# Odd pairs' solve results placed in the other block's PSUM rows

## The chip, the cores and the metric

The kernel runs on one core of one Trainium2 chip. The metric is the device time of one execution in microseconds (us). The core has a matrix engine (TensorE, PE in the profile; its loads of weights are PEld), VectorE (DVE), ScalarE (ACT), GpSimd (POOL), and a sync engine (SP) that issues all the DMA transfers. Results of PE go to PSUM, a small memory of 128 partitions, from which DVE and ACT read them.

## The reference

Two parts follow each other: a recurrent attention over 768 steps for 4 x 8 heads of size 40, and on its output two feed-forward layers.

```
for t in range(S):
    y[:, :, t] = einsum('bhd,bhde->bhe', rt, state)
    Sa = einsum('bhde,bhe->bhd', state, at)
    state = state * wt[:, :, None, :] - einsum('bhd,bhe->bhde', Sa, bt)
    state = state + einsum('bhd,bhe->bhde', vt, kt)
x = y as (3072, 320)
x = ((x @ w1) * (x @ w2)) @ w3 @ w_out        # 320 -> 1024 -> 1024 -> 320
out = (maximum(x @ w_in, 0) ** 2) @ w_out2    # 320 -> 2048 -> 320
```

All is float32.

## The kernel before

**Windows.** The recurrence is cut into chunks of 64 tokens, and within a chunk it becomes matrix algebra. A window n handles one chunk for two of the four batches, 16 heads, so there are 24 windows; even and odd windows belong to different batches. The 16 heads of a window are 8 pairs x (X = 8), and a pair has two heads q = 0 and 1. Head q lies on partitions 64q to 64q + 63 of most tiles.

**The solve.** Within a chunk each token's correction depends on the earlier ones, which is a triangular system of 64 unknown rows per head. It is split in two blocks of BLK = 32 rows. The inverses of the 32x32 diagonal blocks are worked out by POOL, in 31 steps of a multiplication and an addition for all heads at once (`invert`, L660 to L676), and turned by DVE (`turn_inverse`). Then, on PE: `make_u0` (L772) multiplies block 0's inverse with its right-hand side `x_row`; ACT copies the result from PSUM into `uv` (`copy_u`, L1193); `make_x1` (L785) multiplies the block below the diagonal (`n10`) with it; DVE adds the product to block 1 of `x_row` (`add_x1`, L1489); `make_u1` (L798) multiplies block 1's inverse with that; ACT copies again. `turn_uv` (L802) then transposes the complete `uv`.

`make_u0` and `make_u1` both go through `solve_block` (L764). Each batch goes over the 8 pairs and for every x over both q: 16 float32 matmuls, of which the profile lists each twice, as 32. A matmul there has 32 rows, 32 columns of weights and 40 moving columns. The rows of the PE array that it uses follow from the partitions of its operands, the columns from the partitions in PSUM to which its result goes. Results for pair x lie in columns 40x to 40x + 39 of `its_first(n)`, the first half of the PSUM tile `both` (in odd windows of the opening: `aside`), on partitions 64q + 32 at to 64q + 32 at + 31 for block `at`.

**Other steps of a window.** `turn_w`, `turn_ar`, `turn_bk`, `turn_rows` and `turn_uv` are transposes on PE; `cross` (L727), `make_z` (L747), `add_state` (L814), `make_read` (L823), `make_y` (L834) and `turn_state` (L848) are matmuls with up to 128 rows. After each, ACT or DVE takes the result out: `copy_x` and `copy_rows` on ACT, `scan`, `invert_decay` (a reciprocal in two halves), `mask_ak`, `mask_read` and `scale_y` on DVE.

**The experts.** The feed-forward layers run over 6 tiles of 512 tokens. `w3 @ w_out` is multiplied once in the opening (`turn_w3`, `multiply_w3`, on PE between the windows' steps). Weights and activations are split in a high and a low part (`h_hi`, `h_lo`, `x_hi`, `x_lo`), which PE multiplies in 8 terms of 128x512 (`into_hidden`, L866), and in `fold` (L938) and `project` (L953) to the output. For each hidden tile ACT copies one half (`take`), DVE multiplies (`combine`, L1556 or L1558), ACT rounds to `h_hi` (L1250), DVE subtracts to `h_lo` (L1548), and PE awaits `lo_made` before it uses that tile and before it overwrites a bank.

**The order.** It is written out by hand for each engine, with semaphores between them. Windows 0 to 3 (OPENING = 4) lie in an opening that interleaves several windows with the `w3` product. From window 4 on, each engine runs a loop over the windows in which every `next(beside)` stands for one step of the experts; a window has 14 of them, and 56 steps make an expert tile, so that four windows stand beside one expert tile. On PE the order around the change is: `make_u0(n)`, an expert step, `turn_rows(n + 1)`, an expert step, `turn_w(n + 2)`, `make_x1(n)`, an expert step, `make_u1(n)`, an expert step, `turn_uv(n)`. The experts' x of tile i is read back from DRAM (`load_x`) after y of four windows was stored there (`store_y`). After window 23 the last experts run alone.

Of the kernel before, what the change touches and what calls it, by code (L numbers as in the profile page):

```python
# [7 lines left out]
ALU = mybir.AluOpType  # L8
# [69 lines left out]
def attention_with_experts(nc, xT_dram, inputs, w1, w2, w3, w_out, w_in, w_out2, out):  # L78


    P, C, X, DP = 128, inputs.C, inputs.PAIRS, 64
    B, H, S, D = inputs.r.shape
    E = DP + D
    BLK = 32
# [29 lines left out]
    with ExitStack() as ctx:  # L114
        def sb(name, shape, dt=F32):
            return ctx.enter_context(nc.sbuf_tensor(name, shape, dt))
# [4 lines left out]
        w_raw, ar_raw, bk_raw, uv, zv = inputs.w_raw, inputs.ar_raw, inputs.bk_raw, inputs.uv, inputs.zv  # L121
# [14 lines left out]
        invT = [sb(f"invT{h}", [P, X, BLK]) for h in range(2)]  # L136
        x_row = [sb(f"x_row{h}", [P, X, D]) for h in range(2)]
# [79 lines left out]
        def its_both(n):  # L217
            return (aside if n < OPENING and n % 2 else both)[:]

        def its_first(n):  # L220
            return its_both(n)[:, 0:512]
# [10 lines left out]

        def by_head(bank, rows, cols=D):
            return bank[rows, 0:X * cols].rearrange("t (x d) -> t x d", x=X)

        def rbd_of(n):
            return spare[n - 2] if 2 <= n < OPENING else rbd[n % 2]
# [448 lines left out]
        def _(pe):  # L686
# [77 lines left out]
            def solve_block(n, at, signal):  # L764
                for x in range(X):
                    for q in range(2):
                        rows = slice(DP * q + BLK * at, DP * q + BLK * (at + 1))
                        last = nc.tensor.matmul(its_first(n)[rows, x * D:(x + 1) * D], invT[n % 2][rows, x, :], x_row[n % 2][rows, x, :],  # L768
                                                start=True, stop=True)
                last.then_inc(signal, 1)  # L770

            def make_u0(n):  # L772
                pe.wait_ge(inverse_turned, n + 1)
                pe.wait_ge(x_copied, n + 1)
                if n < OPENING - 1:
                    pe.wait_ge(masked_ak, 2 * (n + 3))
                    pe.wait_ge(blocks_copied, 2 * (n + 3))
                elif OPENING <= n and n + 1 < WINDOWS:
                    pe.wait_ge(masked_ak, 2 * (n + 2))
                    pe.wait_ge(blocks_copied, 2 * (n + 2))  # L780
                elif n + 1 == WINDOWS:
                    pe.wait_ge(y_scaled, n)
                solve_block(n, 0, u0_made)

            def make_x1(n):  # L785
                half = n % 2
                pe.wait_ge(u0_copied, n + 1)
                if OPENING <= n and n + 1 < WINDOWS:
                    pe.wait_ge(rows_copied, n + 2)
                for x in range(X):  # L790
                    for q in range(2):
                        lo = DP * q
                        last = nc.tensor.matmul(its_first(n)[lo + BLK:lo + DP, x * D:(x + 1) * D],  # L793
                                                n10[n % 4][lo:lo + BLK, x, :], uv[half][lo:lo + BLK, x, q, 0:D],
                                                start=True, stop=True)
                last.then_inc(x1_made, 1)

            def make_u1(n):  # L798
                pe.wait_ge(x1_added, n + 1)
                solve_block(n, 1, u1_made)  # L800
# [245 lines left out]
            make_u0(0)  # L1046
            turn_ar(3)
            make_x1(0)
            multiply_w3(2, 2)
            multiply_w3(3, 1)  # L1050
# [14 lines left out]
            make_u0(1)  # L1065
            turn_rows(2)
            make_x1(1)
            make_z(2)
            turn_w(4)
# [14 lines left out]
            turn_w(5)  # L1084
            make_z(3)
            make_x1(2)
            multiply_w3(5, 0)
            make_u1(2)
# [73 lines left out]
        def _(act):  # L1162
# [26 lines left out]
            def copy_x(n):  # L1189
                act.wait_ge(z_made, n + 1)  # L1190
                nc.scalar.copy(x_row[n % 2][:], by_head(its_z(n), slice(0, P))).then_inc(x_copied, 1)

            def copy_u(n, at, made, copied):  # L1193
                act.wait_ge(made, n + 1)
                for q in range(2):
                    rows = slice(DP * q + BLK * at, DP * q + BLK * (at + 1))
                    last = nc.scalar.copy(uv[n % 2][rows, :, q, 0:D], by_head(its_first(n), rows))  # L1197
                last.then_inc(copied, 1)

            def reset(n):  # L1200
# [17 lines left out]
            def copy_state(n):  # L1218
                act.wait_ge(turned_state, n + 1)
                nc.scalar.copy(st[n % 2][0:E], by_head(its_second(n), slice(0, E))).then_inc(st_copied, 1)  # L1220
# [98 lines left out]
            for c in range(4):  # L1319
                rows = slice(BLK * c, BLK * (c + 1))  # L1320
                last = nc.scalar.copy(unit_rows[rows], ident[rows, rows].rearrange("i (x r) -> i x r", r=4).unsqueeze(
                    3).broadcast_to([BLK, X, 4, X]))
# [20 lines left out]
            copy_w3(3)  # L1343
            copy_blocks(2)
            copy_u(0, 0, u0_made, u0_copied)
            copy_r(3)
            copy_u(0, 1, u1_made, u1_copied)
            round_fold(2)
            copy_uvT(0)
# [4 lines left out]
            copy_w3(5)  # L1354
            copy_state(0)
            copy_u(1, 0, u0_made, u0_copied)
            copy_rows(2)
            round_split(0)
# [67 lines left out]
        def _(dve):  # L1426
# [62 lines left out]
            def add_x1(n):  # L1489
                dve.wait_ge(x1_made, n + 1)  # L1490
                for q in range(2):
                    rows = slice(DP * q + BLK, DP * (q + 1))
                    last = nc.vector.tensor_tensor(x_row[n % 2][rows], by_head(its_first(n), rows), x_row[n % 2][rows],
                                                   ALU.add)
                last.then_inc(x1_added, 1)

            def new_state(n):
# [153 lines left out]
            fill_lanes(2)  # L1651
            scale_a(3)
            add_x1(0)
            invert_decay(3, 0)
            invert_decay(3, 1)
# [7 lines left out]
            fill_lanes(3)  # L1663
            scale_y(0)
            add_x1(1)
            rest_of_split(0)
            scan(4)
# [9 lines left out]
            fill_lanes(4)  # L1677
            scan(5)
            add_x1(2)
            rest_of_fold(4)  # L1680
            invert_decay(5, 0)
# [57 lines left out]
def attention_then_experts(nc, r, k, v, w, a, b, w1, w2, w3, w_out, w_in, w_out2, out):  # L1739
    B, H, S, D = r.shape  # L1740

    xT_dram = nc.dram_tensor("xT", (H * D, B * S), F32, kind="Internal").ap()
    with ExitStack() as ctx:
        inputs = Inputs(nc, ctx, r, k, v, w, a, b)
        attention_with_experts(nc, xT_dram, inputs, w1, w2, w3, w_out, w_in, w_out2, out)
# [22 lines left out]
```

## Time and profile before

| | us |
|---|---|
| median of 3 runs | 1058.69 (1058.61 to 1059.34) |
| profiled execution | 1060.74 |
| its span | 1059.0 |
| PE busy | 1023.2 (97%) |
| PE, loads of weights | 880.8 (83%) |
| DVE busy | 634.7 (60%) |
| POOL busy | 486.1 (46%) |
| ACT busy | 419.7 (40%) |

The busy times are those of one profiled execution. Loads of weights overlap matmuls. A matmul's end is modelled, so a batch of matmuls overlaps the first one after it by up to 0.2 us in the listing; the starts are what to go by. Times in the text count from the start of the span. The granted clock of PE is full for most of the span, and lower in two stretches before 120 us.

### The profile page before, as it was taken

The page shows a single profiled execution, that of the slowest core. Times are in us where ns is not written, and L with a number is a line of the kernel's source. Part 1 is how long each engine was busy: PE and PEld are TensorE (multiplying, and loading weights), DVE is VectorE, ACT ScalarE, POOL GpSimd, SP SyncE. Part 2 cuts the span into 40 slices and gives each one's busy share as a digit, 9 for nine tenths or more (in the row PEclk, how much of TensorE's full clock was granted, in tenths as well). Part 3 has the DMA queues.
Part 4 walks back from the last instruction along what each step waited for, and adds up shares of the span by engine and source line. Part 5 has one row for each costly group of instructions (what it writes and reads, how often), then busy time and mean ns, then how long its engine had stood idle before and what let it go on. Part 6 is the DMA issues. An engine that isn't in the chain of part 4 may idle for free.

```text
span 1059.0 us, 27606 instructions
## 1 busy us (share of the span) xinstructions
PE 1023.2 (97%) x11008; PEld 880.8 (83%) x11008; DVE 634.7 (60%) x1005; ACT 419.7 (40%) x796; POOL 486.1 (46%) x1573
## 2 busy tenths in 40 slices
PE   5998989999999999999999999999999999999998
PEld 5786768779898888898888898888988888897797
DVE  6876366777875656666567566467567555442333
ACT  3453434454543343443344343334434234332332
POOL 4777755527447346346346355355365364200000
PEclk8997999999999999999999999999999999999999
DMA  9953556756886764757665757756648744555552
GB/s 177 188 127 65 155 132 170 197 165 203 226 234 178 170 150 126 180 145 180 151 157 131 176 140 202 150 134 155 160 125 217 154 117 132 154 169 184 166 170 75
DMA packets 267390, 169.05 MB, mean 160 GB/s; under 512 B 199680, under 2 KB 229376, under 8 KB 267264
## 3 DMA queue, kind: packets, MB, share of 16 engines
q1 hardware_dynamic: 267264, 167.29, 62.7%
q8 instruction: 88, 1.44, 0.6%
q14 instruction: 38, 0.31, 0.1%
HBM read 141.03 MB, written 26.21 MB: 158 GB/s over the span
## 4 chain that ended last, share of the span: by engine, by line
PE 79%; DVE 4%; ACT 2%; issue 1%; ACTq 0%; DVEq 0%
PE aside L866 31%; PE moe_bank L953 16%; PE moe_bank L938 8%; PE both L830 3%; PE both L730 3%; PE both L768 3%; PE both L840 2%; PE both L844 2%; PE both L760 2%; PE both L811 2%; PE both L743 1%; PE both L819 1%; PE both L793 1%; PE both L853 1%; PE both L716 1%
## 5 line engine op out<-in xcount | busy, mean ns | idle before, releaser
L671 POOL TENSOR_TENSOR inv_tmp<-blk,inv 128x60 f32<-128x60 f32 (+24 forms) x744 | 209.5, 282 | 358.4 <-DVE blk L1480 301.4
L675 POOL TENSOR_TENSOR inv<-inv,inv_tmp 128x60 f32<-128x60 f32 (+24 forms) x744 | 237.4, 319 | 58.3
L953 PE MATMUL moe_bank<-v_ring,h_hi 128*128 128x320 f32 x768 | 175.3, 315 | 0.0
L866 PE MATMUL aside<-x2T_hi,w_ring 128*128 128x512 f32 x480 | 148.0, 405 | 4.4 <-DVE h_lo L1548 4.3
L866 PE MATMUL aside<-xT_hi,w_ring 128*128 128x512 f32 x480 | 148.2, 406 | 2.2 <-DVE h_lo L1548 1.5
L1558 DVE SCALAR_TENSOR_TENSOR aside<-aside,left 128x512 f32<-128x512 f32 x96 | 66.9, 697 | 122.0 <-ACT left L1258 122.0
L953 PEld LDWEIGHTS moe_bank<-v_ring,h_hi 128*128 128x128 f32 x768 | 128.0, 188 | 3.9
L1548 DVE TENSOR_TENSOR h_lo<-aside,h_hi 128x512 fp32r<-128x512 f32 x144 | 97.4, 677 | 49.7 <-ACT h_hi L1250 49.0
L1250 ACT CAST h_hi<-aside 128x512 fp32r<-128x512 f32 x144 | 84.7, 588 | 94.9 <-DVE aside L1558 49.6
L953 PE MATMUL moe_bank<-v_ring,h_lo 128*128 128x320 f32 x384 | 118.6, 309 | 0.0
L1258 ACT ACTIVATE left<-aside 128x512 f32<-128x512 f32 x96 | 57.4, 598 | 117.3 <-PE aside L866 117.3
L866 PEld LDWEIGHTS aside<-x2T_hi,w_ring 128*128 128x128 f32 x480 | 84.1, 188 | 21.3 <-issue 6.3
L866 PEld LDWEIGHTS aside<-xT_hi,w_ring 128*128 128x128 f32 x480 | 84.7, 188 | 19.2 <-DVE h_lo L1548 2.6
L866 PE MATMUL aside<-xT_lo,w_ring 128*128 128x512 f32 x288 | 97.1, 391 | 0.0
L866 PE MATMUL aside<-x2T_lo,w_ring 128*128 128x512 f32 x288 | 96.9, 391 | 0.0
L1438 DVE RECIPROCAL undecay<-decay 104x256 f32<-104x256 f32 x48 | 83.2, 1739 | 0.2
L938 PE MATMUL moe_bank<-h_hi,v_ring 128*128 128x512 f32 x240 | 81.4, 404 | 0.0
L953 PEld LDWEIGHTS moe_bank<-v_ring,h_lo 128*128 128x128 f32 x384 | 72.1, 188 | 0.0
L1556 DVE TENSOR_TENSOR aside<-left,aside 128x512 f32<-128x512 f32 x48 | 33.0, 687 | 63.1 <-PE aside L866 63.1
L866 PEld LDWEIGHTS aside<-xT_lo,w_ring 128*128 128x128 f32 x288 | 54.1, 188 | 12.8 <-DVE xT_lo L1564 0.6
L866 PEld LDWEIGHTS aside<-x2T_lo,w_ring 128*128 128x128 f32 x288 | 54.1, 188 | 12.3 <-DVE x2T_lo L1586 0.2
L1197 ACT COPY uv<-both 32x320 f32<-32x320 f32 x88 | 36.8, 418 | 68.9 <-PE both L768 63.4
(151 smaller groups left out, 1604.2 us busy)
## 6 DMA issues: line engine op xcount, KB each, us to landing
w_ring<-gate_rows SPq DMA_DIRECT2D x40, 640.0 KB, 4.6
w_ring<-win_rows SPq DMA_DIRECT2D x40, 640.0 KB, 4.1
v_ring<-wout_rows SPq DMA_DIRECT2D x80, 320.0 KB, 3.1
v_ring<-fold_rows SPq DMA_DIRECT2D x48, 320.0 KB, 4.2
gate_rows<-w_ring SPq DMA_DIRECT2D x8, 640.0 KB, 6.4
win_rows<-w_ring SPq DMA_DIRECT2D x8, 640.0 KB, 4.4
wout_rows<-v_ring SPq DMA_DIRECT2D x16, 320.0 KB, 5.9
stage<-in_moe_w SPq DMA_DIRECT2D x8, 512.0 KB
```

Source lines behind the costliest of these rows:

```text
L671: nc.gpsimd.tensor_tensor(tmp, x[:, j, 0:j].unsqueeze(2).broadcast_to([P, j, X - lo]), mine[:, j:j + 1, lo:X].broadcast_to([P, j, X - lo]) ...
L675: nc.gpsimd.tensor_tensor(mine[:, 0:j, lo:X], mine[:, 0:j, lo:X], tmp, ALU.add).then_inc(solve, 1)
L866: last = nc.tensor.matmul(bank(use), w, x, start=n == 0, stop=n == len(terms) - 1)
L938: last = nc.tensor.matmul(bank(f"x{m}"), weights[:, lo:lo + P], h[at % RING][:], start=f == 0 and n == 0, stop=f == FT - 1 and n == len(te ...
L953: last = nc.tensor.matmul(bank(f"o{s}")[:, 0:M], h[at % RING][:, s * P:(s + 1) * P], weights[:, rest * M:(rest + 1) * M], start=f == 0 and ...
L1197: last = nc.scalar.copy(uv[n % 2][rows, :, q, 0:D], by_head(its_first(n), rows))
L1250: nc.scalar.copy(h_hi[at % RING][:], hidden_at(x)).then_inc(hi_made, 1)
L1258: nc.scalar.activation(left[x % 2][:], hidden_at(x), ACT.Relu).then_inc(taken, 1)
L1438: nc.vector.reciprocal(undecay[0:E, xs], decay[n % 4][0:E, xs, 1:C + 1]).then_inc(undecayed, 1)
L1548: nc.vector.tensor_tensor(h_lo[at % RING][:], hidden_at(x), h_hi[at % RING][:].bitcast(F32), ALU.subtract).then_inc(lo_made, 1)
L1556: nc.vector.tensor_tensor(into, left[x % 2][:], into, ALU.mult).then_inc(combined, 1)
L1558: nc.vector.scalar_tensor_tensor(out=into, in0=into, scalar=0.0, in1=left[x % 2][:], op0=ALU.max, op1=ALU.mult).then_inc(combined, 1)
```

## The change

Results of the three batches for odd pairs (x odd) go to the other block's partitions in PSUM: for block `at`, to 64q + 32 (at ^ 1). Even pairs stay. Operands stay where they are. In PSUM, then, a block's results of even pairs and of odd pairs lie on different partitions, and each reader takes them in two instructions, one for the even and one for the odd pairs, each with half the pairs: `copy_u` on ACT has four copies of 32 x 160 for two of 32 x 320, `add_x1` on DVE four additions for two. The destination in `uv` and `x_row` is as before. Semaphores, waits and order don't change.

```diff
--- before.py
+++ after.py
@@ -232,6 +232,13 @@
 
         def by_head(bank, rows, cols=D):
             return bank[rows, 0:X * cols].rearrange("t (x d) -> t x d", x=X)
+
+        def solved_rows(q, at, odd):
+
+            return slice(DP * q + BLK * (at ^ odd), DP * q + BLK * ((at ^ odd) + 1))
+
+        def solved(n, q, at, odd):
+            return by_head(its_first(n), solved_rows(q, at, odd))[:, odd::2, :]
 
         def rbd_of(n):
             return spare[n - 2] if 2 <= n < OPENING else rbd[n % 2]
@@ -765,8 +772,8 @@
                 for x in range(X):
                     for q in range(2):
                         rows = slice(DP * q + BLK * at, DP * q + BLK * (at + 1))
-                        last = nc.tensor.matmul(its_first(n)[rows, x * D:(x + 1) * D], invT[n % 2][rows, x, :], x_row[n % 2][rows, x, :],
-                                                start=True, stop=True)
+                        last = nc.tensor.matmul(its_first(n)[solved_rows(q, at, x % 2), x * D:(x + 1) * D],
+                                                invT[n % 2][rows, x, :], x_row[n % 2][rows, x, :], start=True, stop=True)
                 last.then_inc(signal, 1)
 
             def make_u0(n):
@@ -790,7 +797,7 @@
                 for x in range(X):
                     for q in range(2):
                         lo = DP * q
-                        last = nc.tensor.matmul(its_first(n)[lo + BLK:lo + DP, x * D:(x + 1) * D],
+                        last = nc.tensor.matmul(its_first(n)[solved_rows(q, 1, x % 2), x * D:(x + 1) * D],
                                                 n10[n % 4][lo:lo + BLK, x, :], uv[half][lo:lo + BLK, x, q, 0:D],
                                                 start=True, stop=True)
                 last.then_inc(x1_made, 1)
@@ -1194,7 +1201,8 @@
                 act.wait_ge(made, n + 1)
                 for q in range(2):
                     rows = slice(DP * q + BLK * at, DP * q + BLK * (at + 1))
-                    last = nc.scalar.copy(uv[n % 2][rows, :, q, 0:D], by_head(its_first(n), rows))
+                    for odd in range(2):
+                        last = nc.scalar.copy(uv[n % 2][rows, odd::2, q, 0:D], solved(n, q, at, odd))
                 last.then_inc(copied, 1)
 
             def reset(n):
@@ -1490,8 +1498,9 @@
                 dve.wait_ge(x1_made, n + 1)
                 for q in range(2):
                     rows = slice(DP * q + BLK, DP * (q + 1))
-                    last = nc.vector.tensor_tensor(x_row[n % 2][rows], by_head(its_first(n), rows), x_row[n % 2][rows],
-                                                   ALU.add)
+                    for odd in range(2):
+                        mine = x_row[n % 2][rows, odd::2, :]
+                        last = nc.vector.tensor_tensor(mine, solved(n, q, 1, odd), mine, ALU.add)
                 last.then_inc(x1_added, 1)
 
             def new_state(n):
```

## Rows read from the trace of the kernel before

**Rows 1.** The page: busy time (share, instructions), and the chain by engine.
```profile
PE 1023.2 (97%) x11008; PEld 880.8 (83%) x11008; DVE 634.7 (60%) x1005; ACT 419.7 (40%) x796; POOL 486.1 (46%) x1573
...
PE 79%; DVE 4%; ACT 2%; issue 1%; ACTq 0%; DVEq 0%
```

**Rows 2.** Stretches: start:end, length, busy (instructions) of each engine, PE clock, DMA share, GB/s.
```profile
79.00:100.00 21.00, 16.04 (x256) 14.27 (x257) 13.89 (x19) 6.72 (x14) 16.56 (x57) 0.88 0.42 75
300.00:460.00 160.00, 159.51 (x1791) 138.72 (x1786) 100.34 (x158) 64.64 (x124) 78.69 (x261) 1.00 0.67 165
```

**Rows 3.** Timeline of PE in window 13: start, us, line, operation, count.
```profile
519.99 0.39 PE L866 MATMUL aside<-xT_lo,w_ring 128*128 128x512 f32 x1
520.31 0.76 PE L768 MATMUL both<-x_row,invT 32*32 32x40 f32 x32
521.00 0.50 PE L938 MATMUL moe_bank<-h_hi,v_ring 128*128 128x512 f32 x1
...
526.91 1.20 PE L866 MATMUL aside<-xT_hi,w_ring 128*128 128x512 f32 x4
...
528.95 0.76 PE L768 MATMUL both<-x_row,invT 32*32 32x40 f32 x32
```

**Rows 4.** Groups of PE: line, tile, shape, count, busy us, mean ns, idle before.
```profile
L830 PE MATMUL both<-rbd,uvT 104*128 104x128 f32 x352 | 42.9, 275 | 0.0
L768 PE MATMUL both<-x_row,invT 32*32 32x40 f32 x1408 | 34.6, 202 | 6.6 <-DVE azk L1471 6.3 <-DVE x_row L1493 0.3
...
L760 PE MATMUL both<-zv,azk 128*64 128x40 f32 x352 | 25.1, 233 | 0.9 <-ACT bk_row L1187 0.9
...
L853 PE MATMUL both<-ident,sT 104*40 104x40 f32 x640 | 15.7, 206 | 0.0
```

**Rows 5.** Timeline of PE, batches of other steps.
```profile
535.04 1.11 PE L760 MATMUL both<-zv,azk 128*64 128x40 f32 x32
...
538.03 1.95 PE L830 MATMUL both<-rbd,uvT 104*128 104x128 f32 x16
...
543.58 0.78 PE L853 MATMUL both<-ident,sT 104*40 104x40 f32 x32
```

**Rows 6.** Groups of ACT: copies by shape.
```profile
L1197 ACT COPY uv<-both 32x320 f32<-32x320 f32 x88 | 36.8, 418 | 68.9 <-PE both L768 63.4 <-issue 3.4
...
L1182 ACT COPY n<-both 32x256 f32<-32x256 f32 x44 | 16.0, 363 | 15.7 <-DVE azk L1471 15.4
...
L1284 ACT COPY third<-moe_bank 64x512 f32<-64x512 f32 x6 | 3.5, 585 | 13.0 <-PE moe_bank L938 13.0
```

**Rows 7.** Groups of DVE: additions and multiplications by shape.
```profile
L1471 DVE TENSOR_TENSOR azk<-both,above 64x512 f32<-64x512 f32 x44 | 30.3, 689 | 1.0
...
L1493 DVE TENSOR_TENSOR x_row<-both,x_row 32x320 f32<-32x320 f32 x44 | 21.6, 490 | 25.8 <-PE both L793 25.1
```

**Rows 8.** Timeline of DVE in window 16, from add_x1.
```profile
648.11 0.99 DVE L1493 TENSOR_TENSOR x_row<-both,x_row 32x320 f32<-32x320 f32 x2 [1.24 <-PE both L793]
...
651.19 1.74 DVE L1438 RECIPROCAL undecay<-decay 104x256 f32<-104x256 f32 x1
652.85 0.63 DVE L1548 TENSOR_TENSOR h_lo<-aside,h_hi 128x512 fp32r<-128x512 f32 x1
```

**Rows 9.** Timeline of PE in window 16, the expert step after turn_uv.
```profile
653.53 1.20 PE L866 MATMUL aside<-xT_hi,w_ring 128*128 128x512 f32 x4
```

**Rows 10.** Timeline of PE in the opening; idle time before it in brackets.
```profile
96.96 1.27 PE L768 MATMUL both<-x_row,invT 32*32 32x40 f32 x32 [4.29 <-DVE azk L1471]
```

**Rows 11.** Timeline of DVE in the opening.
```profile
93.72 0.67 DVE L1486 STREAM_TRANSPOSE invT<-inv 128x256 f32<-128x256 f32 x1 [4.71 <-POOL inv L675]
```

**Rows 12.** Groups of ACT between 118 and 146 us.
```profile
L1265 ACT CAST xT_hi<-x_raw 128x512 fp32r<-128x512 f32 x3 | 1.7, 618 | 4.3 <-DMA x_raw<-xT 4.3
```

## Prediction

> **What bounds the kernel now.** I read the page first: TensorE (PE) is busy 97% of the span and the chain that ended last is 79% PE [rows 1]. The table by stretch then says where this holds. From 300 us on PE is busy 159.51 of 160 us at full clock, with VectorE (DVE) at 100 and ScalarE (ACT) at 65; between 79 and 100 us it is busy only 16.04 of 21 us, at a mean clock of 0.88 [rows 2]. So a microsecond taken from PE's instructions in the steady stretch (windows 4 to 23) shortens the kernel, unless a wait takes its place; in the opening (windows 0 to 3) it may be lost to an idle stretch.
>
> The order of PE's work there shows what the change touches: a solve, then a step of the expert matmuls, which covers the reply of ACT or DVE [rows 3]. Each window has three such batches (two solves at L768, one product at L793), so 72 batches, 60 of them in windows 4 to 23. The code has 16 float32 matmuls in a batch and the profile 32; every one of them stands twice (as do the 8 of L830, listed as 16). "A matmul" below is such a record.
>
> **What one batch costs, and what sets it.** A batch runs from its first start to its last end in 0.76 us [rows 3]; one matmul lasts 202 ns in the mean [rows 4]. So 31 starts lie in about 0.56 us: one every 18.2 ns. Records of the two head parities q already lie in different tiles of the array (rows 0 and columns 0, rows 64 and columns 64). One tile thus gets a matmul every 36.4 ns. Is that the tile's own speed? The read step, a single stream of 128 columns, takes (1.95 - 0.275)/15 = 112 ns each, 0.87 ns a column [rows 4, 5]; 40 columns are then 35 ns. That fits 36.4, and it says that a tile streams at full speed and that the two tiles overlap completely. turn_state (L853) has 104 rows in both parities, so its two tiles share all rows and differ in columns alone, and its spacing is (0.78 - 0.206)/31 = 18.5 ns [rows 4, 5]: two column tiles over the same rows overlap as well as two disjoint ones. That is the case the change makes: even pairs keep their columns, odd pairs go to the other 32, and four column tiles are in use, each row group feeding two, as in L853.
>
> **PE, the gain.** If four overlap, each tile still takes 36.4 ns a matmul, now four per period: one start every 9.1 ns. The batch shrinks by 31 x 9.1 = 0.28 us; I take 0.27, since the first loads are exposed either way. Bounds: nothing (the spacing stays 18.2) to 0.28. Below nothing: if the load of weights into one column tile can't run beside a matmul of the neighbour on the same rows. make_z, with 64 weight columns and 40 moving ones, has (1.11 - 0.233)/31 = 28.3 ns [rows 4, 5], 57 ns in a tile, so a load costs 0.88 ns a column, 28 ns for 32 columns; exposed for each pair it would add 16 x 28 = 0.45 us to a batch (16 matmuls in each of the two tiles). I take a value near the upper end, because L853 and L760 overlap both loads and matmuls over shared rows. The number of PE instructions and their waits stay.
>
> The Trainium skill ("TensorE: Matmul & The Clock Gate", section "The mechanism") says that a weight load overlaps running matmuls only when the row group differs. L853's rows above disagree for two tiles of 64 columns; for neighbours of 32 columns no row shows it. By that rule the change would bring nothing on PE, and perhaps the loss just bounded. The same page ("Wait — 56ns, not 53.3ns?") states a least start-to-start of about 25 ns; the 18.2 ns of these rows are below it, so I don't let it bound the new spacing.
>
> **ACT and DVE, the cost.** copy_u becomes four copies of 32x160 for two of 32x320. 256 columns take 363 ns and 512 take 585 [rows 6], 0.87 ns a column; 160 columns come to 280. Extra: 4 x 280 - 2 x 418 = 0.28 us, twice a window. That the odd copy reads other partitions than it writes should cost nothing: the copy of L1284 reads rows 64 to 127 into 0 to 63 and is on this same line. add_x1: 512 columns 689 ns, 320 490 [rows 7], so 160 are 324, and four come to 0.32 us more than two. Between-instruction gaps are nearly nothing on both engines. Every-second-head reads could cost more; bounds: from 0.28 and 0.32 down to 0 and up to a doubling.
>
> Where are they covered? After x1 PE has an expert step of 2.04 us (526.91 to 528.95) before the second solve [rows 3], while add_x1 takes 0.99 us; 1.32 still fits. The same step covers copy_u. One place in four windows isn't covered. In windows 4, 8, 12, 16 and 20 DVE goes without a pause from add_x1 through the scan, a combine and a reciprocal to the h_lo that PE's next expert step awaits: 648.11 to 653.48 [rows 8], and PE starts at 653.53 [rows 9]. From x1 to there DVE sets the time. The gain of the second solve (0.27) is swallowed and 0.32 is added: 5 x 0.59 = 3.0 us. DVE's other chains start after cross or the state steps, far from add_x1. Windows 22 and 23, where DVE's combine comes late, and the crowded part before 300 us get an allowance of 1.0 us.
>
> **The opening.** PE idles 4.29 us before the first solve of window 2, and reports DVE's azk [rows 10]; DVE itself sat 4.71 us until the inverse from GpSimd (POOL) was there [rows 11]. POOL's chain of inversions doesn't change, so windows 0 and 1 gain nothing; their slower copies vanish in the same idle time. Window 2 then runs at half clock, 1.27 us a batch [rows 10], and would save about 0.5 three times. Window 3 saves 0.81 but has hardly any cover (one small multiply of 1.3 us): about 0.55 goes back. 1.5 + 0.3 = 1.8 us. They pass on, because the experts start when x is loaded from the y just stored (ACT waits 4.3 us on that DMA) [rows 12]. Bounds 0 to 3.
>
> **Sum.** 60 x 0.27 = 16.2; less 3.0; less 1.0; plus 1.8: 14.0 us. The profiled execution took 1060.74 us (span 1059.0), so 1046.7 in its terms; the median of the runs is 2.05 below it: 1044.7, rounded to 1045 (-1.3%).
>
> **The rivals.** *Half the overlap.* Something shared by the four (the supply of 64 loads and matmuls in 0.28 us, half the time it has now) stops the spacing near 13.6 ns. For: nothing in the trace runs denser than 18.2. Against: it would have to bind just below what is seen. The same terms as in the sum are then 60 x 0.14 - 5 x (0.14 + 0.32) - 0.7 + 1.0 = 6.4: 1052 us. Chance 0.14.
> *It doesn't do what it says.* Neighbouring columns on one row group take turns, PE is unchanged, and the longer add_x1 shows five times (1.6 us), in the opening about 1: 1061 us, on the edge of what can be told. Chance 0.13.
> *Slower: exposed weight loads.* The 0.45 us above in 72 batches, 32 us plus the 2.6: about 1093 us. It decides as soon as over 4 ns per matmul are added. Against: shared rows overlap in L853. Chance 0.05.
> *The forecast*, four tiles at once: 0.66, with its own range of 1040 to 1049. The last 0.02 is for a clock loss in the opening or unforeseen.
>
> **How the numbers follow.** About 0.2% (2 us) can be told from no change. Faster: 0.66 + 0.14 + a bit of the second rival = 0.81. Same: 0.08, from the second rival. Slower: 0.11, its other half and the third. The range reaches from all 72 batches gaining with few waits (1039) to past the half overlap: 1056.
>
> **What would show it.** L768 and L793 batches of about 0.49 us from first start to last end, for 0.76; PE's step from a solve to the next expert step 0.42 for 0.69; ACT's copies 280 ns, twice as many; DVE's adds 324 ns; a stall before the expert step after turn_uv in one window of four, with h_lo as its releaser; the idle time before 97 us longer by up to 1.6. Batches of 0.76 or more prove the forecast wrong; so do batches of 0.49 with new PE waits of over 5 us in the steady stretch.

## The result and the profile after

| | before | changed |
|---|---|---|
| median of 4 runs | 1058.76 us | 1046.43 us (1045.58 to 1049.25) |
| profiled execution, span | 1059.0 us | 1047.5 us |
| PE busy | 1023.2 us | 1005.5 us |
| ACT busy, instructions | 419.7 us, 796 | 432.0 us, 892 |
| DVE busy, instructions | 634.7 us, 1005 | 641.1 us, 1053 |

The ratio is 0.9882 (95% interval 0.9860 to 0.9904). Measured again in a later session, beside three of the experiments (run changed_again), it was 0.9888 (0.9868 to 0.9907; 1046.04 us for 1059.29). The forecast was 1045 us.

The page of the changed kernel, against [rows 1]:

```profile
span 1047.5 us, 27750 instructions
...
PE 1005.5 (96%) x11008; PEld 860.6 (82%) x11008; DVE 641.1 (61%) x1053; ACT 432.0 (41%) x892; POOL 485.4 (46%) x1573
...
PE 75%; DVE 7%; issue 2%; ACT 2%; ACTq 0%; DVEq 0%
```

PE lost 17.7 us of work, and its share of the chain that ended last went from 79% to 75%, DVE's from 4% to 7%. The stretch from 300 us, against [rows 2] (columns as there):

```profile
300.00:460.00 160.00, 159.12 (x1829) 137.80 (x1828) 102.26 (x167) 66.78 (x141) 78.84 (x262) 1.00 0.66 163
```

PE stays all but full, so what it saves there is time. PE's timeline in window 16, against [rows 3]:

```profile
633.91 0.39 PE L873 MATMUL aside<-xT_lo,w_ring 128*128 128x512 f32 x1
634.23 0.49 PE L775 MATMUL both<-x_row,invT 32*32 32x40 f32 x32
634.65 1.20 PE L873 MATMUL aside<-xT_hi,w_ring 128*128 128x512 f32 x4
...
639.87 0.49 PE L800 MATMUL both<-uv,n 32*32 32x40 f32 x32
640.28 1.19 PE L873 MATMUL aside<-xT_hi,w_ring 128*128 128x512 f32 x4
...
642.32 0.49 PE L775 MATMUL both<-x_row,invT 32*32 32x40 f32 x32
642.74 1.19 PE L873 MATMUL aside<-xT_hi,w_ring 128*128 128x512 f32 x4
...
644.70 1.03 PE L818 MATMUL both<-ident,uv 128*104 128x128 f32 x8
646.18 1.19 PE L873 MATMUL aside<-xT_hi,w_ring 128*128 128x512 f32 x4 [0.45 <-DVE h_lo L1557]
```

A batch lasts 0.49 us for 0.76, and from a solve's first start to the next expert step there are 0.42 us for 0.69. The last line carries what was lost: the expert step after turn_uv finds PE idle for 0.45 us, and names h_lo (by the starts it is 0.69 us late: 1.48 us after turn_uv, for 0.79 in the windows where nothing waits and 0.86 here in the kernel before). The groups of PE, against [rows 4]; one matmul lasts as long as before, so the whole gain is in how many run at once:

```profile
L775 PE MATMUL both<-x_row,invT 32*32 32x40 f32 x1408 | 22.2, 203 | 6.9 <-DVE azk L1479 5.0 <-DVE x_row L1503 1.9
...
L800 PE MATMUL both<-uv,n 32*32 32x40 f32 x704 | 11.0, 203 | 0.0
```

ACT's and DVE's new readers, against [rows 6] and [rows 7]:

```profile
L1205 ACT COPY uv<-both 32x160 f32<-32x160 f32 x176 | 49.7, 282 | 56.5 <-PE both L775 54.9
```

```profile
L1503 DVE TENSOR_TENSOR x_row<-both,x_row 32x160 f32<-32x160 f32 x88 | 28.3, 321 | 21.0 <-PE both L800 19.7
```

The steady stretch can be read off far more exactly than the total: the first solve of window 12 to that of window 16, which is one expert tile's period. Before it is 161.70 us (in the same timeline the starts are 479.69 and 641.39). The changed kernel:

```profile
475.17 0.49 PE L775 MATMUL both<-x_row,invT 32*32 32x40 f32 x32
...
634.23 0.49 PE L775 MATMUL both<-x_row,invT 32*32 32x40 f32 x32
```

159.06 us, 2.64 less, and the same in each later group of four windows, to 0.01 us. The experiments below are read by this period, since the totals scatter by several microseconds from chip to chip and run to run (24 runs of the kernel before on one chip lie between 1055.97 and 1063.6). What the starts are inside one batch is told in ns from the first (PE's records in one batch of L768 or L775; for each of the 16 matmuls two of them):

```
before : 0 6 52 59 93 100 129 136 165 ...          566   (565 or 566 in 46 of 48 batches, the others at half clock)
changed: 0 6 13 20 52 59 65 72 93 100 106 113 ...  292   (292 or 293 in 45 of 48, the others in the opening)
```

Two starts per period of 36 ns, 6 to 7 ns apart, have become four, 6.5 ns apart.

### The profile page after: what moved, and what is told of

Same layout as the page of the kernel before. It is cut to its first block, busy times and chain, and to the rows that moved or that the text cites. A ratio compares the mean times of both kernels' runs of the same rounds, so it can differ in the third digit from the quotient of the medians.

```text
span 1047.5 us, 27750 instructions
## 1 busy us (share of the span) xinstructions
PE 1005.5 (96%) x11008; PEld 860.6 (82%) x11008; DVE 641.1 (61%) x1053; ACT 432.0 (41%) x892; POOL 485.4 (46%) x1573
## 4 chain that ended last, share of the span: by engine, by line
PE 75%; DVE 7%; issue 2%; ACT 2%; ACTq 0%; DVEq 0%
PE aside L873 30%; PE moe_bank L960 15%; PE moe_bank L945 8%; PE both L837 3%; PE both L737 3%; PE both L847 2%; PE both L851 2%; PE both L767 2%; PE both L775 1%; PE both L826 1%; PE both L818 1%; PE both L750 1%; PE both L860 1%; PE both L723 1%; PE both L707 1%
## 5 line engine op out<-in xcount | busy, mean ns | idle before, releaser
L1205 ACT COPY uv<-both 32x160 f32<-32x160 f32 x176 | 49.7, 282 | 56.5 <-PE both L775 54.9
L873 PEld LDWEIGHTS aside<-x2T_lo,w_ring 128*128 128x128 f32 x288 | 54.1, 188 | 12.3 <-DVE x2T_lo L1595 0.2
```

The source lines that it names most:

```text
L873: last = nc.tensor.matmul(bank(use), w, x, start=n == 0, stop=n == len(terms) - 1)
L1205: last = nc.scalar.copy(uv[n % 2][rows, odd::2, q, 0:D], solved(n, q, at, odd))
```

## Experiments

The diffs are against the changed kernel, with lines left out.

**split_only.** Is it the overlap of column tiles, or do the split reads do something?

```diff
-            return slice(DP * q + BLK * (at ^ odd), DP * q + BLK * ((at ^ odd) + 1))
+            return slice(DP * q + BLK * at, DP * q + BLK * (at + 1))
```

> The readers are split in even and odd pairs as in the changed kernel (four copies of 32x160, four additions), but the results stay in their old PSUM rows. Theory (the gain is the overlap of four column tiles): batches stay at 0.76 us, PE gains nothing, only the cost of the split is left: h_lo later by 0.32 us in five windows (1.6 us) and about 1 us in the opening, so about 1061 us. Rival (the split itself frees something, or costs more than the sums say): 1050 or less, or 1064 or more.

Measured: 1060.86 us for 1061.06 of the kernel before on that chip, 0.9991 (0.9974 to 1.0008), so no difference against the kernel before on its own chip. The expected 1061 us was met in the number alone: it stood for a loss of 2.3 us, and the interval goes from 2.8 us faster to 0.8 slower, so a loss of that size is ruled out. The batches are 0.76 us:

```profile
477.54 0.76 PE L775 MATMUL both<-x_row,invT 32*32 32x40 f32 x32
...
639.41 0.76 PE L775 MATMUL both<-x_row,invT 32*32 32x40 f32 x32
```

The period is 161.87 us, 0.17 longer than before and not 0.32. The reason stands in add_x1, which took 1.14 us here and 1.33 in the changed kernel (next two fences, DVE's timelines in window 16, split_only and then the changed kernel):

```profile
646.12 1.14 DVE L1503 TENSOR_TENSOR x_row<-both,x_row 32x160 f32<-32x160 f32 x4 [1.24 <-PE both L800]
```

```profile
640.42 1.33 DVE L1503 TENSOR_TENSOR x_row<-both,x_row 32x160 f32<-32x160 f32 x4 [0.99 <-PE both L800]
641.78 1.56 DVE L1438 TENSOR_TENSOR_SCAN decay<-both,zeros 104x64 f32<-104x64 f32 x8
643.25 0.67 DVE L1565 TENSOR_TENSOR aside<-left,aside 128x512 f32<-128x512 f32 x1
643.84 1.74 DVE L1446 RECIPROCAL undecay<-decay 104x256 f32<-104x256 f32 x1
645.50 0.63 DVE L1557 TENSOR_TENSOR h_lo<-aside,h_hi 128x512 fp32r<-128x512 f32 x1
```

The instructions last the same, 318 and 320 ns in the median. But their starts differ (ns from the first; DVE's additions, ACT's copies):

```
split_only: DVE 0 245 564 819     ACT 0 190 481 675
changed:    DVE 0 330 657 1002    ACT 0 294 586 882
```

Where two instructions in a row read the same PSUM rows, the second starts 72 ns (DVE) or 93 ns (ACT) before the first ends. In the changed kernel each reads other rows than the last, and starts 12 to 14 ns after its end. So the split itself is cheaper than forecast, and the move of rows takes this back.

**evens_first, twos, evens3.** How far does PE look for a free tile? The three differ from the changed kernel in the order of pairs alone.

```diff
-                for x in range(X):
+                for x in [*range(0, X, 2), *range(1, X, 2)]:      # evens_first
+                for x in (0, 2, 1, 3, 4, 6, 5, 7):                # twos
+                for x in (0, 2, 4, 1, 3, 5, 6, 7):                # evens3
```

> As the changed kernel, but each batch runs over pairs 0, 2, 4, 6 and then 1, 3, 5, 7, so that the four column tiles are never asked for in turn. Theory A (matmuls start in program order and one whose tile is busy holds back all behind it): two tiles at a time, batches of 0.76 us, and the time of split_only, about 1061 us. Theory B (PE picks any matmul of its queue whose tile is free): batches of 0.49 us and 1046 us.

> As the changed kernel, with pairs in the order 0, 2, 1, 3, 4, 6, 5, 7. In evens_first the first odd pair started just when pair 4 did, with pair 6's two matmuls still waiting for their tiles: PE seems to look past one waiting pair (two matmuls), not past more. Theory (a look-ahead of one pair): pair 1 goes past the waiting pair 2, full overlap, batches of 0.49 us. Rival (a fixed time or a start-up effect, no look-ahead): pair 1 waits until pair 2 has started, batches of 0.56 us or more.

> As the changed kernel, with pairs in the order 0, 2, 4, 1, 3, 5, 6, 7. Theory (a look-ahead of one pair): pair 1 can't pass two waiting pairs (2 and 4) and starts with pair 2, one pair's time (73 ns) late, batches of 0.49 + 0.07 = 0.56 us. Rival (it looks past two pairs and more): 0.49 us. With the order of evens_first the same rule gives two pairs' time, 0.49 + 0.15 = 0.64 us, measured 0.65.

Measured: evens_first 1055.37 us, 0.9946 (0.9930 to 0.9963); twos 1049.74 and evens3 1050.56 us in one run each, beside 1061.83 of the kernel before. The first solves of windows 12 and 16, in this order (periods of 160.80, 159.33 and 160.07 us):

```profile
476.76 0.65 PE L775 MATMUL both<-x_row,invT 32*32 32x40 f32 x32
...
637.56 0.65 PE L775 MATMUL both<-x_row,invT 32*32 32x40 f32 x32
```

```profile
474.87 0.51 PE L775 MATMUL both<-x_row,invT 32*32 32x40 f32 x32
...
634.20 0.51 PE L775 MATMUL both<-x_row,invT 32*32 32x40 f32 x32
```

```profile
473.60 0.58 PE L775 MATMUL both<-x_row,invT 32*32 32x40 f32 x32
...
633.67 0.58 PE L775 MATMUL both<-x_row,invT 32*32 32x40 f32 x32
```

evens_first refuted both theories: 0.65 us is neither 0.76 nor 0.49. The starts say why (ns from the first; the odd pairs' first start in brackets, told from the spacing: the even pairs' tiles take a new start only every 36 ns):

```
changed    : 0 6 [13] 20 52 59 65 72 ...                        292
twos       : 0 7 [27] 34 53 59 79 86 94 100 ...                 313
evens3     : 0 7 53 60 94 100 [106] 113 130 ...                 385
evens_first: 0 7 52 59 93 100 129 136 165 172 [177] 184 ...     457
```

With one waiting pair ahead of it the first odd pair starts almost at once, 27 ns into the batch; with two ahead it waits until one of them has started; with three, until two have. Each pair more costs 72 ns, a pair's time in a tile. So PE goes past one waiting pair (two matmuls), not past two. The expectation of evens3 (0.56) was met at 0.58 and that of twos (0.49) at 0.51; the rule itself was made from evens_first, so that its 0.64 for the 0.65 there is a fit and not a forecast. What these orders can't tell apart is a look-ahead of one pair from a strict order of issue in which each tile holds one waiting matmul beside the running one: both give the same four rows. Why the 27 ns in twos are not 13 isn't settled (the odd tile's first load starts at 25 ns there and at 12 in the changed kernel).

A version with q crossed instead (an odd pair's head 0 on head 1's rows, so that two row groups meet in one column tile) wasn't tried, so nothing here says whether two row groups overlap in one column tile.

**solves_only and x1_only.** What is each batch worth? In the first only `solve_block` and `copy_u` are changed, in the second only `make_x1` and `add_x1`.

```diff
# solves_only: make_x1 and add_x1 as before
-                        last = nc.tensor.matmul(its_first(n)[solved_rows(q, 1, x % 2), x * D:(x + 1) * D],
+                        last = nc.tensor.matmul(its_first(n)[lo + BLK:lo + DP, x * D:(x + 1) * D],
# x1_only: solve_block and copy_u as before
-                        last = nc.tensor.matmul(its_first(n)[solved_rows(q, at, x % 2), x * D:(x + 1) * D],
+                        last = nc.tensor.matmul(its_first(n)[rows, x * D:(x + 1) * D],
```

> Only the two solves put odd pairs in the other rows; make_x1 and add_x1 are as before. Theory (each batch is worth 0.274 us, but in one window of four the second solve's gain is lost to DVE's chain from add_x1): four windows take 161.70 - 8 x 0.274 + 0.27 = 159.8 us; 0.990 of the kernel before. Rival (all batches count alike and the chain doesn't matter): 159.5 or less.

> Only make_x1 and add_x1 are changed; solves and ACT's copies are as before. Theory (4 batches of 0.274 gained, 0.34 us lost once in four windows, since DVE's four additions take 1.32 us for 0.98 and the chain passes this on): 161.70 - 1.10 + 0.34 = 160.9 us for four windows, 0.997 of the kernel before. Rival (the loss is hidden): 160.6.

Measured: 1048.41 us, 0.9907 (0.9889 to 0.9924), and 1057.44 us, 0.9985 (0.9970 to 1.0000).

```profile
473.63 0.49 PE L775 MATMUL both<-x_row,invT 32*32 32x40 f32 x32
...
633.45 0.49 PE L775 MATMUL both<-x_row,invT 32*32 32x40 f32 x32
```

```profile
478.48 0.76 PE L775 MATMUL both<-x_row,invT 32*32 32x40 f32 x32
...
639.41 0.76 PE L775 MATMUL both<-x_row,invT 32*32 32x40 f32 x32
```

Periods of 159.82 and 160.93 us, where the theory had 159.8 and 160.9 and the rivals 159.5 and 160.6; the rivals fall. The gains, 1.88 and 0.77, sum to 2.65, the changed kernel's 2.64. make_x1's four batches are thus worth 0.77 us a period and not 1.10.

**late_recip, late_recip_old.** Is the rest of the loss DVE's chain? In windows 4, 8, 12, 16 and 20 the first half of the reciprocal comes one step later, in the changed kernel and in the one before.

```diff
                 next(beside)
-                if two:
+                if two and n % 4:
                     invert_decay(n + 2, 0)
                 next(beside)
+                if two and n % 4 == 0:
+                    invert_decay(n + 2, 0)
                 if two:
                     invert_decay(n + 2, 1)
```

> As the changed kernel, but in windows 4, 8, 12, 16 and 20 DVE runs the first half of the reciprocal one expert step later, behind the h_lo that PE awaits. Theory (in these windows DVE's chain from add_x1 sets PE's time; PE starts that expert step at 646.18 and could at 645.49 in window 16): h_lo no longer stalls PE there, 5 x 0.69 = 3.4 us less than the changed kernel, about 1043 us. Rival (the delayed reciprocal pushes the state or the y of the window and PE waits there): same as the changed kernel, 1046 us, with a wait for state_tmp, x_row or ruv in the place of h_lo's.

> The same move of the reciprocal in the kernel before. Theory: there PE's expert step started 0.07 us late by h_lo, so 5 x 0.07 = 0.3 us at most, 1058.4 us: the stall is one that the change made. Rival (the place was already a full stall): over 2 us less.

Measured: late_recip 1042.40 us, 0.9824 (0.9792 to 0.9856); late_recip_old 1058.91 us, 0.9980 (0.9961 to 0.9999).

```profile
470.17 0.49 PE L775 MATMUL both<-x_row,invT 32*32 32x40 f32 x32
...
628.50 0.49 PE L775 MATMUL both<-x_row,invT 32*32 32x40 f32 x32
```

```profile
477.57 0.76 PE L768 MATMUL both<-x_row,invT 32*32 32x40 f32 x32
...
639.16 0.76 PE L768 MATMUL both<-x_row,invT 32*32 32x40 f32 x32
```

The period falls by 0.73 to 158.33 us in the changed kernel, as its theory has it, and by 0.11 to 161.59 in the one before, where 0.07 was expected: the stall is one that the change made. The old kernel's total fell by more, 2.1 us with an interval from 0.1 to 4.1, than five times 0.11. By the total alone the rival (over 2 us less) would stand; it is the period that refutes it for the steady windows. The rest of the 2.1 us lies outside them, and I can't tell it from the scatter. DVE in window 16 of late_recip, h_lo now ahead of the reciprocal and waiting for ACT alone:

```profile
634.69 1.32 DVE L1503 TENSOR_TENSOR x_row<-both,x_row 32x160 f32<-32x160 f32 x4 [0.99 <-PE both L800]
...
638.96 0.69 DVE L1557 TENSOR_TENSOR h_lo<-aside,h_hi 128x512 fp32r<-128x512 f32 x1 [0.76 <-ACT h_hi L1258]
639.57 1.74 DVE L1446 RECIPROCAL undecay<-decay 104x256 f32<-104x256 f32 x1
```

PE's waits for h_lo, in the kernel before (300 to 925 us), the changed kernel and late_recip (300 to 900 us each; engine, line, for what: us in total, times, longest):

```profile
PE aside L866 <- DVE h_lo L1548: 2.0, 4, 0.5
```

```profile
PE aside L873 <- DVE h_lo L1557: 3.5, 8, 0.4
```

```profile
PE aside L873 <- DVE h_lo L1557: 1.8, 4, 0.5
```

The four waits of the kernel before stand at another expert step (before x2T_hi, one per period), and stay in all three; the change added four, and late_recip has lost these. After turn_uv of windows 12, 16 and 20 the next start comes 0.86 us later in the kernel before, 1.48 in the changed one and 0.79 in late_recip.

late_recip is the fastest version here. Its interval and those of the changed kernel (0.9860 to 0.9904, 0.9868 to 0.9907) don't overlap, though they come from different sessions; the periods leave no doubt. Five times 0.73 us are 3.65, and the medians lie 3.6 and 4.0 us apart. By the ratios to the kernel before it would be 6 to 7 us; the part beyond 3.65 isn't explained, and the scatter of the kernel before on that chip is as large. With the reciprocal late in both, the change is worth 161.59 - 158.33 = 3.26 us a period, which is 12 batches of 0.272.

**steady_only, changed_again.** What does the opening bring? steady_only has rows, copies and additions of windows 0 to 3 as before; changed_again is the changed kernel.

```diff
-        def solved_rows(q, at, odd):
+        def solved_rows(n, q, at, odd):
+            odd = odd if n >= OPENING else 0
```

> The changed kernel once more, as the measure for the three kernels beside it and for the one with the late reciprocal: 0.988 of the kernel before, four windows in 159.06 us (161.70 before).

> The change in windows 4 to 23 alone; windows 0 to 3 are as before, reads unsplit. Theory (the opening's gain, 3.7 us at window 4, is nearly gone by window 8, where the changed kernel is only 1.9 us ahead, since a DMA for the weights and a stretch of half clock take it): within 2 us of the changed kernel. Rival (the opening's batches are a real part of the gain): 3 to 4 us slower than the changed kernel. Four windows take 159.06 us in both.

Measured beside each other: 1046.04 (0.9888) and 1048.98 us (0.9914, 0.9898 to 0.9931), 2.9 us apart; the four runs of one (1045.44 to 1046.73) and of the other (1048.69 to 1049.78) don't overlap. The period of steady_only is 159.07 us, as in the changed kernel. My theory, that less than 2 us of the opening's gain last, falls; the figure is near the rival's 3 to 4. It had leaned on one profiled execution, the changed kernel's first, which lost time after window 4: from window 4 to window 8 it took 169.75 us, for 167.94 in the kernel before and 166.12 in changed_again. One loss is in window 7: ACT's copy of the second solve stood behind a rounding that awaited a DMA, and PE waited 2.44 us (ACT's and PE's timelines, changed kernel):

```profile
285.37 0.46 ACT L1247 CAST v_ring<-stage 128x320 fp32r<-128x320 f32 x1 [3.58 <-DMA stage<-in_moe_w_out]
285.85 1.16 ACT L1205 COPY uv<-both 32x160 f32<-32x160 f32 x4
```

```profile
287.12 1.05 PE L818 MATMUL both<-ident,uv 128*104 128x128 f32 x8 [2.44 <-issue]
```

The other is the granted clock. Around window 2 the kernel before was at half clock from 94.9 to 108.6 us, the changed one from 98.6 to 105.4 (stretches as in [rows 2]; first before, then changed):

```profile
94.90:98.60 3.70, 1.64 (x36) 1.58 (x37) 3.63 (x4) 1.71 (x4) 2.92 (x11) 0.50 0.00 0
98.60:105.40 6.80, 6.80 (x97) 5.24 (x97) 4.54 (x12) 2.16 (x5) 5.47 (x18) 0.50 0.09 30
105.40:108.60 3.20, 3.20 (x24) 2.19 (x21) 1.76 (x2) 0.83 (x2) 2.57 (x9) 0.50 0.55 162
```

```profile
94.90:98.60 3.70, 2.16 (x74) 2.01 (x74) 3.67 (x7) 2.52 (x7) 2.91 (x11) 1.00 0.15 27
98.60:105.40 6.80, 6.80 (x79) 4.44 (x77) 5.96 (x13) 2.79 (x7) 5.39 (x18) 0.50 0.25 75
105.40:108.60 3.20, 3.18 (x45) 2.31 (x44) 0.51 (x2) 1.01 (x1) 2.57 (x9) 0.99 0.67 248
```

The changed kernel then had 3.4 us at half clock after 146.4. Where such stretches fall isn't the same in two executions of one kernel: changed_again had them, beside the one near 20 us that all have, at 98.3 and 139.3, each 3.4 us. Over the twelve traces two things can be told apart. The stretch that begins between 94 and 99 us is 3.4 us long in changed_again and 6.8 in the five others with all three batches changed in the opening; it is 10.2 us in split_only, solves_only and steady_only, and 13.7 in the kernel before, late_recip_old and x1_only. So its length goes with the change. The later stretch of 3.4 us comes in six of the twelve (at 285 us in twos, between 139 and 151 in the others), steady_only and x1_only among them, so it doesn't go with the change.

## Why the prediction was right

**Four column tiles overlap: shown.** The batch was to shrink by 0.27 us and shrank by 0.273 (566 to 292.5 ns between first and last start). The key step was to read turn_state's batch as two column tiles over shared rows [rows 4, 5]; the four-tile case differs from it only in the number of columns. split_only shows that nothing else of the change does it. (The column tile and the PSUM rows to which it writes go together, and no run here tells one from the other.) The rivals of half overlap, none, and exposed loads are all out. The prediction said against itself that nothing in the trace runs denser than a start every 18.2 ns. That holds of the mean alone: the starts in the kernel before stand in pairs, 6 to 7 ns apart, and so do those of turn_state. Loads for neighbouring column tiles of one row group start 13 ns apart in the changed kernel, beside running matmuls, and a tile takes a record every 36 ns, less than the 28 of its load and the 35 of its columns together (both worked out in the prediction). So the rule of the Trainium skill ("TensorE: Matmul & The Clock Gate", section "The mechanism") that a load overlaps running matmuls only when the row group differs doesn't hold here. The same section also lets a load go ahead into a background weight buffer, and with that the traces agree.

**The readers: right per instruction, off in the gaps.** 280 and 324 ns were forecast for 282 and 321. I put the gaps at nothing and bounded the whole between 0 and a doubling. add_x1 takes 0.34 us more than before for 0.32; the rest are two more gaps of 13 to 14 ns. That instructions which read the same rows overlap, as split_only showed, was not in the forecast, and the forecast comes out because the changed kernel's don't.

**One window in four isn't covered: shown.** 0.59 us was forecast; the period gives 12 x 0.273 - 2.64 = 0.64 us. late_recip takes this stall away, 0.73 us with the 0.11 that was there before.

**The other terms of the sum.** The allowance of 1.0 us for windows 22 and 23 and for the part before 300 us was too small, as far as single traces can say. From the first solve of window 20 to the end the changed kernel took 254.22 us for 255.91, 1.7 us less, where 12 batches and one stall give 2.6. In windows 22 and 23 DVE starts add_x1 late, behind a combine, and the second solve starts right behind it; solves_only, with the shorter add_x1, took 254.02 there. From window 4 to window 8 it was 166.12 (changed_again) for 167.94, 1.8 for 2.6. Part of that is window 4, where the second solve also starts right behind add_x1, 3.41 us after make_x1 for 3.10 before. Together 1.7 us were lost for the 1.0. But this stretch differs more between executions than the term is large: 169.75 in the changed kernel's first trace, and 167.33 in split_only. So the 0.9 us at the end are measured, and the 0.8 are those of one pair of executions. The opening was put at 1.8 us and is worth 2.9. That the two errors, 0.7 too much and 1.1 too little, nearly cancel is luck. The sum took window 2's three batches to stay at half clock; in the changed kernel the first of them ran before the clock fell, and the stretch at half clock was half as long. That the 1.1 us are all due to this is argued, not shown. One recorded sign didn't come either: PE's idle time before window 2's first solve was to grow by up to 1.6 us and fell, to 3.03 us for 4.29 [rows 10]. Why stays open.

```profile
96.44 0.57 PE L775 MATMUL both<-x_row,invT 32*32 32x40 f32 x32 [3.03 <-DVE azk L1479]
```

**The total.** 14.0 us were forecast, 12.3 and 13.3 measured, in two comparisons. I had taken the profiled execution's 2.05 us over the median as a constant cost of the profile. It isn't: changed_again's profiled execution was below its median (1045.44 to 1046.04). Differences of two single traces, 11.5 and 15.4 us here, say less than the medians.

## What to carry to other kernels

Small matmuls whose outputs need only 32 partitions can be spread over all four column tiles by choosing the PSUM partitions of their results. Here, from two tiles to four, the time from the first to the last start halved (566 to 292 ns), with no instruction more on PE; it takes that neighbours in program order ask for different tiles. Before counting the gain, follow what the readers' extra instructions stand ahead of on their own engine: one place in four windows cost a fifth of it here, and moving one long instruction behind the one that PE awaited brought that back. In a kernel with a period, measure the period in the trace: it told 0.1 us apart where totals told 2.

## What the runs showed of the hardware

- Four column tiles over two row groups take float32 matmuls of 32 rows, 32 weight columns and 40 moving columns at once: a start every 36 ns in each tile, 6.5 ns apart between tiles, as fast per tile as with two tiles.
- PE passes over a waiting pair of matmuls for one whose column tile is free (or holds one waiting matmul in each tile), but not over two pairs: 292, 313, 385 and 457 ns from first to last start with none, one, two and three in front.
- An instruction on DVE or ACT that reads the same PSUM rows as the one before it starts 72 or 93 ns before that one's end; with other rows it starts 12 to 14 ns after it. That is 0.19 us in four additions of 32x160 and 0.21 us in four copies.
- The half-clock stretches in the opening differ from one execution to the next of the same kernel, in place and in length (6.8 and 3.4 us near 98 us in two executions of the changed kernel), but by less than with the change: 3.4 to 6.8 us in the six traces with all of it in the opening, 10.2 to 13.7 in the six without.
